# Attention, soft experts and sorted experts on one core: the weight stage in a new order

## The reference

```python
q_s = softmax(q, axis=-1); k_s = softmax(k, axis=2)          # attention
x = q_s @ (k_s.T @ v)                                         # per batch and head
logits = x @ phi                                              # 4608 x 32
d = softmax(logits, axis=0); slot_input = d.T @ x             # 32 x 512
for e in range(8):                                            # four slots each
    slot_out[e] = relu(slot_input[e] @ w1[e]) @ w2[e]         # w1 512x1024, w2 1024x512
x = softmax(logits, axis=1) @ slot_out                        # c @ slot_out
e_idx = argmax(x @ w_gate, axis=1)                            # second mixture
out[n] = gate_w[n] * sigmoid(x @ w_output_gate)[n, e] * (relu(x[n] @ v1[e]) @ v2[e])   # e = e_idx[n]
```

## Time and profile before

| | |
|---|---|
| median of three runs | 594.95 us |
| the profiled execution | 595.87 us, span 594.1 us |
| mean granted TensorE clock | 0.876 of full |
| busy, share of span | PE 73%, DVE 56%, ACT 38%, POOL 37% |
| DMA | 106.75 MB, mean 180 GB/s |
| chain that ended last | PE 50%, DVE 19%, ACT 11%, issue 8%, DMA 6%, POOL 3% |

### The profile page before, as it was taken

One profiled execution on the slowest core, in us unless ns is written; L12 is line 12 of the kernel. 1 busy time (PEld: TensorE's weight loads), 2 busy tenths in 40 slices (PEclk: granted clock), 3 DMA queues, 4 the chain that ended last, 5 costly groups with the idle time before them and its releaser, 6 DMA issues.

```text
span 594.1 us, 12702 instructions
## 1 busy us (share of the span) xinstructions
PE 436.5 (73%) x4552; PEld 255.0 (43%) x4553; DVE 335.0 (56%) x546; ACT 223.9 (38%) x327; POOL 221.3 (37%) x142
## 2 busy tenths in 40 slices
PE   1588988897774455640087739999999999999931
PEld 0466766675453233510022314545545455454420
DVE  4889999963363340676969753334344343443552
ACT  0356767665235556493522421212122121121220
POOL 2355555552005528095600032343332433423341
PEclk9989999989797686755579969999999999999955
DMA  9949999446898399963549400111111111111000
GB/s 309 379 131 375 384 384 382 169 168 239 281 393 324 142 377 394 389 248 124 202 159 394 156 6 24 54 55 39 56 51 43 56 38 56 55 39 54 35 19 1
DMA packets 44854, 106.75 MB, mean 180 GB/s; under 512 B 4560, under 2 KB 5648, under 8 KB 44816
## 3 DMA queue, kind: packets, MB, share of 16 engines
q1 hardware_dynamic: 37888, 95.42, 43.2%
q0 software_dynamic: 4816, 10.06, 5.2%
q10 hardware_dynamic: 2112, 0.71, 0.5%
HBM read 96.25 MB, written 11.88 MB: 182 GB/s over the span
## 4 chain that ended last, share of the span: by engine, by line
PE 50%; DVE 19%; ACT 11%; issue 8%; DMA 6%; POOL 3%; SPq 0%; DVEq 0%; POOLq 0%; ACTq 0%
PE banks L1477 32%; PE banks L1464 3%; DVE big L781 3%; ACT big L641 3%; DMA big<-in_k 3%; PE banks L1347 3%; DMA kvg<-in_moe_w 2%; PE banks L1413 2%; DVE top L916 2%; DVE big L754 2%; DVE big L767 2%; PE banks L1335 2%; PE banks L1205 1%; POOL big L491 1%; POOL big L504 1%
## 5 line engine op out<-in xcount | busy, mean ns | idle before, releaser
L1477 PE MATMUL banks<-big,work 128*128 x864 | 193.8, 382 | 0.6 <-ACT work L739 0.6
L1477 PEld LDWEIGHTS banks<-big,work 128*128 128x128 f16 x864 | 83.3, 98 | 95.4 <-issue 2.7
L739 ACT ACTIVATE work<-banks 128x512 f16<-128x512 f32 x86 | 46.8, 595 | 188.4 <-PE banks L1464 188.4
L1112 DVE TENSOR_SCALAR work<-banks,tok,unscale 128x512 f32<-128x512 f32 x43 | 34.8, 810 | 129.6 <-PE banks L1477 126.7
L519 POOL DMA_INDIRECT out<-work,token_of x43 | 43.6, 1015 | 139.8 <-DVE split_ct L1094 129.4
L512 POOL DMA_INDIRECT tok<-token_rows,token_of x43 | 44.0, 1023 | 62.8 <-issue 56.7
L504 POOL TENSOR_TENSOR big<-kvg,big 128x2048 f16<-128x2048 f32 x8 | 32.4, 4071 | 86.6 <-ACT kvg L643 86.6
L1104 DVE SCALAR_TENSOR_TENSOR work<-banks,work 128x512 f16<-128x512 f32 x86 | 55.2, 684 | 3.8 <-ACT work L739 3.8
L491 POOL TENSOR_TENSOR big<-big 128x1152 f32<-128x1152 f32 x16 | 33.5, 2117 | 58.1 <-DVE big L786 58.1
L1171 PE MATMUL banks<-big 64*64 64x128 f32 x1152 | 36.5, 279 | 7.4 <-ACT big L546 6.0
L754 DVE TENSOR_REDUCE big<-big 128x256 f32<-128x2304 f32 x8 | 34.1, 4258 | 8.6 <-DMA big<-in_k 8.6
(11 more groups left out here) (217 smaller groups left out, 658.7 us busy)
## 6 DMA issues: line engine op xcount, KB each, us to landing
ring<-in_moe_w SPq DMA_DIRECT2D x14, 2048.0 KB, 14.1
big<-in_moe_w SPq DMA_DIRECT2D x10, 2048.0 KB, 14.5
big<-in_k SPq DMA_DIRECT2D x8, 1152.0 KB, 6.6
big<-in_q SPq DMA_DIRECT2D x8, 1152.0 KB, 7.3
big<-in_v SPq DMA_DIRECT2D x8, 1152.0 KB, 9.6
kvg<-in_moe_w SPq DMA_DIRECT2D x8, 1024.0 KB, 8.6
big<-in_moe_w SPq DMA_DIRECT2D x6, 1024.0 KB, 10.6
ring<-in_moe_w SPq DMA_DIRECT2D x2, 1024.0 KB, 13.4
```

The costliest lines, as they stand in the source:

```text
L739: act.activation(h_hi[n][:, b * 512:(b + 1) * 512], psum[2 * n + b], ACT.Relu).then_inc(h_hi_ready, 1)
L1112: dve.tensor_scalar(y_out[n], psum[4 + n], srt[:, ds(t, 1), NS], unscale[:, ds(ev, 1)], ALU.mult, ALU.mult).then_inc(y_scaled, 1)
L1477: return pe.matmul(psum[4 + n], h[n][:, j * P:(j + 1) * P], w_pair[:, ds(ev, 1), w, j, :].rearrange("p o n -> p (o n)"), start=j == 0 and ...
```

## The change

The outputs are computed by the same steps. The parts:

1. **Buffers and loads.** A table `HELD` gives each of seven 2 MB buffers the matrices that it holds one after the other; v2 now uses big_4, big_5, big_6, big_7, ring_a, ring_b and kvg. SP's list has a new order, and one half of v2's second matrix is loaded during attention.
2. **Order.** The functions of a slot expert are cut into steps (slot_h, turn_hid, slot_o, turn_res; keep_hid, keep_hidT, keep_res, keep_out), those of v2 into w_max, spread_w, w_scale, w_hi, w_raw, w_low by half, those of g into g_max, spread_g, g_scale, g_hi, g_low, and every engine's list mixes them step by step.
3. **Scales.** The bits of the exponent are inverted by one instruction in place of max, mask, reciprocal and product; the small floor comes in through one more PSUM column.
4. **Small operands of the routing** (sums, positions, tile numbers) lie in PSUM, not in SBUF, and one addition is merged.
5. **Moved:** row softmax's shift, product and low part go from DVE to POOL; nine constant or index instructions of DVE go from the middle stage to the start of attention.

```diff
-            def scale_of(e, goal, spread_done, spread_tops, step, low_pow, dst):
-                dve.tensor_reduce(out=top_all[:, :], in_=spread_tops, axis=X, op=ALU.max).then_inc(step, 1)
-                dve.tensor_scalar(low_pow, top_all[:, :], TINY, None, ALU.max).then_inc(step, 1)
-                dve.tensor_scalar(bits, bits, 0x7F800000, None, ALU.bitwise_and).then_inc(step, 1)
-                dve.reciprocal(dst, low_pow).then_inc(step, 1)
-                dve.tensor_scalar(dst, dst, goal, None, ALU.mult).then_inc(step, 1)
...
+            def scale_of(at_, tops, step, count, dst, done):
+                dve.tensor_reduce(out=top_all[:, at_:at_ + 1], in_=tops, axis=X, op=ALU.max).then_inc(step, 1)
+                dve.wait_ge(step, count)
+                dve.tensor_scalar(dst.bitcast(I32), top_all[:, at_:at_ + 1].bitcast(I32), BITS, BITS, ALU.bitwise_and,
+                                  ALU.bitwise_xor).then_inc(done, 1)
...
+        HELD = dict(
+            b4=(("w1", 6),),
+            b5=(("v2", 1), ("w1", 7), ("v2", 6),),
+            b6=(("w1", 0), ("w1", 4), ("v2", 3),),
+            b7=(("w2", 0), ("v2", 2), ("w2", 6),),
+            kv=(("v2", 0), ("w2", 5), ("w2", 7), ("v2", 7),),
+            ra=(("w1", 1), ("w2", 4), ("v2", 5), ("v1", 1), ("v1", 3), ("v1", 5), ("v1", 7),),
+            rb=(("w2", 1), ("w1", 5), ("v2", 4), ("v1", 0), ("v1", 2), ("v1", 4), ("v1", 6),))
...
             sp.wait_ge(slot_in_done, 1)
-            load_v2(1)
+            load_half(1, 0)
+            sp.wait_ge(slot_o_done, 1)
+            load_v2(2)
             sp.wait_ge(slot_h_done, 1)
-            load(big_6, w1, 4, m6_loaded)
...
+            load_w1(4)
             sp.wait_ge(slot_o_done, 2)
-            load(ring_b, w2, 5, b_loaded)
+            load_w1(5)
+            sp.wait_ge(slot_h_done, 5)
+            load_v2(3)
+            load_w2(4)
+            sp.wait_ge(slot_h_done, 6)
+            load_v2(4)
+            sp.wait_ge(slot_o_done, 4)
+            load_w1(6)
             sp.wait_ge(w_split, 2)
-            load_v2(2)
+            load_w2(5)
             sp.wait_ge(w_split, 4)
-            load_v2(3)
...
+            load_w1(7)
...
+            def c_low():
+                pool.wait_ge(c_hi_done, 2)
+                pool.tensor_tensor(rows16[:, :, NS:2 * NS], logit, rows16[:, :, 0:NS], ALU.subtract).then_inc(c_lo_done, 1)
...
             dve.tensor_copy(steps_f[:, :], steps).then_inc(steps_done, 1)
+            dve.memset(gate_bd[:, :, :], 0.0).then_inc(fold_step, 1)
+            dve.wait_ge(ids_made, 1)
+            dve.tensor_scalar(id_part, pos[:, :], 6, None, ALU.logical_shift_right).then_inc(ids_split, 1)
...
             dve.wait_ge(consts_ready, 6)
...
-                dve.tensor_copy(pos[:, :], row_a[:, :]).then_inc(pos_step, 1)
-            dve.tensor_scalar(pos_t[:, :], pos[:, :], 7, None, ALU.logical_shift_right).then_inc(pos_g, 1)
...
+                dve.tensor_copy(pos_i, row_pos).then_inc(pos_step, 1)
+                dve.tensor_scalar(pos_t, pos_i, 7, None, ALU.logical_shift_right).then_inc(pos_g, 1)
...
+            def g_hi(e):
+                n = e % 2
+                act.wait_ge(g_scaled, e + 1)
+                if e == 0:
+                    act.wait_ge(w_split, 16)
...
+            set_gates()
+            w_max(7, 1)
+            choose()
+            factor()
+            set_places()
+            w_scale(7)
```

More of the change, by code:

```diff
@@ L17 @@
 EPS = 1e-9
-TINY = 1e-30
+TINY = 2.0 ** -100
 C_SCALE = 2.0 ** 7
-G_TOP = 2.0 ** 7
-W_TOP = 2.0 ** 14
+TOP = 7
+BITS = 0x7F800000
 SKIP = 1 << 20
@@ L726, in _ @@
+            w_raw(6, 1)
             keep_parts(0)
-            w_hi(7, 2 * E - 4)
+            w_hi(7, 0)
+            w_raw(7, 0)
+            w_hi(7, 1)
             keep_parts(1)
-            for e in range(E):
-                g_hi(e, e % 2)
-                if e + 2 < E:
-                    keep_parts(e + 2)
+            w_raw(7, 1)
+            keep_parts(2)
+            g_hi(0)
+            store_table()
+            g_hi(1)
+            keep_parts(3)
+            keep_parts(4)
+            g_hi(2)
@@ new lines, in _ @@
+            w_max(6, 0)
+            w_max(6, 1)
+            w_max(7, 0)
+            w_scale(6)
+            set_gates()
[4 more added lines that the diff above has]
+            w_scale(7)
+            one_hots(0)
+            g_max(0)
+            g_scale(0)
+            w_back()
+            g_max(1)
+            g_scale(1)
+            g_low(0)
+            one_hots(1)
+            g_max(2)
+            g_low(1)
+            g_scale(2)
+            one_hots(2)
@@ L1400, in project @@
+            def project(e):
+                src, done, number = held("v1", e)
+                pe.wait_ge(done[0], number)
+                if e:
                     pe.wait_ge(g_parts_kept, e)
@@ new lines, in _ @@
+            turn_c(0, 6)
+            turn_c(1, 7)
+            turn_c(2, 5)
+            spread_w(3)
+            turn_res(2)
+            slot_h(6)
+            turn_hid(5)
+            slot_o(4)
+            turn_res(3)
+            spread_w(4)
+            slot_o(5)
+            turn_hid(6)
+            slot_h(7)
+            turn_res(4)
+            slot_o(6)
+            turn_res(5)
+            turn_hid(7)
+            spread_w(5)
+            turn_res(6)
+            slot_o(7)
+            turn_res(7)
@@ L1454, in turn @@
+            fold_up(7)
+            find_tokens(3)
+            spread_g(7)
             def turn(t, n, reused=True):
```

919 lines of the change are left out of this document (555 added, 364 removed).

## The result

| | before | after |
|---|---|---|
| median of four runs | 594.73 us (593.52 to 595.52) | 570.58 us (569.95 to 571.80) |
| the profiled execution | 595.87 us, span 594.1 | 569.95 us, span 568.2 |
| mean granted TensorE clock | 0.876 | 0.886 |

The ratio is 0.960 (95% interval 0.9575 to 0.9622): 24 us faster. Forecast were 565 us, with 554 to 581 as the range.

The account below looks back on a forecast made before the run. The prediction took the middle stage's chain of waits, with the DMA queue partly idle, as the bound. The loop starting 33.7 us earlier and attention's +3.5 gave -30.2, so 565 us; 8-in-10 range 554 to 581.

Parts of the forecast that it names:

- Attention, forecast +3.5: Attention's start: id_part waits for POOL's q_shift(0), k_max(1) at 23.0 instead of 19.44; +3.5 us, none recovered later.
- Rival 1: Attention's start: no wait, the nine small VectorE instructions slip in or need no ports; 561.5 us, chance 0.18.
- The DMA queue without a gap, last v2 at 242.5: Middle stage: no gap beyond 1.5 us, last v2 half lands at 242.5 instead of being issued at 259.5.
- the walk: Step-by-step timing from w2(3)'s load to take(0), using durations of before and 34.6 MB at 392 GB/s, 88.3 us.
- The margins of 5 to 10 us: Middle stage: w_split 2, 4 and 6 come at 194, 204.5 and 216, each some 5 to 10 us early.
- row softmax on POOL at nothing: Middle stage: c_shift, c_norm, c_low cost nothing, since slot_h(6) waits for w1(6) until 205; without that cover 2.3 us.
- rival 2: Middle stage: order too tight, engines stand behind waiting keeps and the DMA queue drains as before; 580 us, chance 0.18.
- Gates to the end of w_scale(7), forecast 16.7 us after the gates: Routing: gate copies end at 243.9; choose 3.9, factor and exp 1.7, set_places 7.0 us; w_scale(7) done at 260.6.
- -8.5 us for operands in PSUM: Routing, set_places: two instructions held 2.6 and 5.2 us and a third 1.3 take 0.2 each with PSUM operands; -8.5 us.
- POOL's end and g_hi(0): End of the v2 split: POOL ends at 273.4 instead of 295.4, after which g_hi(0) starts at 274.2.
- The g stage, forecast 39.7: g matrices: 34.7 us of VectorE work plus 5.7 of waits; first g_hi to take(0) 39.7 us instead of 41.7.
- rival 4: Tile loop: TensorE enters at the low clock; if it stays at 1.2 GHz for eight tiles, 607 us; chance 0.04.

Follow-up runs that it names:

- v2_waits: Changed kernel with SyncE issuing v2(3) and v2(4) only behind w_split 2 and 4, about as with two v2 buffers: 592.10 us, ratio 0.9949.
- old_order_psum: Kernel before, in its old order, with only the routing's row sums and positions moved to PSUM: 587.84 us, ratio 0.9876.
- rowsum_early: Changed kernel with row softmax's sum earlier on VectorE, its product on POOL ahead of the first low part, turn_res(2) ahead of turn_c: 570.31 us, ratio 0.9586.
- routing_sbuf: Changed kernel, new order, with the routing's sums, positions and their parts back in SBUF: 570.32 us, ratio 0.9575.
- scale_padded: Changed kernel with three more dependent one-column instructions in each of 16 scales, five steps instead of two: 573.62 us, ratio 0.9633.
- gap_filled: Changed kernel with row-softmax, constants and w_scale(7) moved earlier, turn_res(2) before turn_c, w2(4) before slot_h(4)'s wait, w_scale(3) before v2(4)'s maxima: 561.31 us, ratio 0.9419.

## Why the prediction was right or wrong, point by point

The mechanism was right in the main. The gain lies in the middle stage; most of it comes with the v2 loads, whose last half landed 17.1 us earlier (18.9 when attention's 1.8 us are taken off), and v2_waits shows that nearly nothing is left when two of them are late again; the terms of attention, the routing and the g stage have the right sign. The forecast was 5.6 us too low. Times below are in the clock of before; for the kernel after I take off the 1.8 us by which attention ended later (slot_in at 158.63 against 156.86).

- **Attention, forecast +3.5: +1.8 in the profiled execution.** The wait was there, 4.03 us at the second TENSOR_SCALAR instead of `id_part`, and `k_max(1)` came at 22.48 against 23.0. Rival 1 is out for the kernel, though what it says did happen to `id_part`, which slipped through in 0.12 us. What failed is "nothing behind gives it back": 1.2 us came back within attention. Whether the +1.8 is a loss against before these traces can't say, since the old order gave 158.28 in old_order_psum.
- **The DMA queue without a gap, last v2 at 242.5: this is the step that failed, by 6 us.** By the walk the first half of v2(7) lands 2.6 us before the second, at 239.9; its maximum started on landing at 247.71, which is 245.9. (The second landed at 251.0, which is 249.2.) The walk multiplied the bytes by 392 GB/s, the rate of full stretches, and allowed one gap of 1.5 us. From 152 to 250 us it moved 355 GB/s in the mean, and 98 us at 355 instead of 392 are 9.2 us; 2.6 of them are the first window, before w2(3) starts, so 6.6 remain where I had allowed 1.5. By their rates the window at 184 lacks 1.8 us and those from 216 to 228 lack 2.1; the rest is spread over windows with a share near 1 and 311 to 350 GB/s. At 184 slot_h(4) ended 1.9 us late (w1(4) went out at 168.4 and landed at 182.2), and w1(5) was nearly in by then. The margins of 5 to 10 us were used up too. w_split 2 and 4 came 3.7 and 3.9 us later than forecast: ScalarE left its wait for `keep_hidT(3)` at 186.68, which is 184.9, and not at 181.3, since turn_hid(3) stands in TensorE's list behind slot_h(4) and a spread_w. slot_h(7) came 5.0 us late and w_split 6 5.8. I had costed row softmax on POOL at nothing with the cover that slot_h(6) waits for w1(6) anyway. The cover held but for 1.1 us; what was late was the load itself, in at 211.4, which is 209.6, where I had 205. The walk had also missed that ScalarE's `keep_res(3)` stands behind turn_res(2), turn_c and POOL's product, but rowsum_early, which takes that wait away, gained nothing: w1(6) was not in earlier. A queue that runs low behind fixed lists is rival 2's mechanism, at a third of its price.
- **Two slips in the sums.** A window filled to 303/392 leaves 0.9 of its 4 us idle, not 0.7. And g matrices at the pace of before would, by the 41.7 us named there, have brought take(0) at 274.2 + 41.7 = 315.9, not at the 317.6 of the bound. Neither changes the forecast by more than 0.2 us.
- **Gates to the end of w_scale(7), forecast 16.7 us after the gates: 15.9** (251.2 to 267.1). gate_logits took 4.10 as in the earlier trace rows, choose and factor 5.0 against 5.6, set_places with w_scale(7) 6.8 against 7.0. The result was right and one reason was wrong. I had set -8.5 us for operands in PSUM; routing_sbuf shows that in the new order they are worth nothing that could be measured, since POOL happened to be idle there, and old_order_psum that they would have been worth 7 to 8 us in the old.
- **POOL's end and g_hi(0)**, forecast 273.4 and 274.2: 278.4 and 279.1. Both are the delay of 5.5 us with which the gates' copies ended (249.4 against 243.9), less the 0.8 that the routing gave back.
- **The g stage, forecast 39.7: 40.1.** By scale_padded VectorE's list is on its path for part of it.
- **The loop** took 0.7 us more; its first tile's products took 7.5 us and not 6.83. The next were back at 5.18, so rival 4 had no substance.
- **From span to median**, forecast 1.1 us: 2.4, since this execution was 1.8 over its span and the median 0.6 over that.

The sum: 5.3 from the loads to the loop's start, 0.7 in the loop, 1.3 from span to median, less 1.7 in attention is 5.6.

The Trainium skill (SBUF — State Buffer, section "Who interferes with whom") puts a VectorE instruction with two SBUF inputs under the same lock as a copy, cast or tensor_scalar. The kernel old_order_psum agrees: L1060 took 4.24 us beside POOL, and in the kernel after, with POOL idle, the same form took 0.56. The Trainium skill (SBUF — State Buffer, section "A bandwidth-pool intuition that's wrong (but worth ruling out)") gives about 358 GB/s from HBM to one core. The mean of 355 in the kernel after would fit; but gap_filled held 371 over the same 98 us, and windows of 4 us show up to 424. By that figure the walk's 34.6 MB would have been an estimated 96.6 us instead of 88.3, and the forecast 573.
